# Two matmul blocks and an attention block on one core: gate and value of the last 1536 tokens by seven half-size products

## The chip, the cores and the metric

One core of a Trainium2 chip runs the whole program. The metric is device time in microseconds (us) of one execution; lower is better. The four compute engines are TensorE (PE in the profile), VectorE (DVE), ScalarE (ACT) and GpSimd (POOL); SyncE (SP) issues nearly all DMAs. Each engine works through its own instructions in order and waits for the others by semaphores.

## The reference

```python
kv = np.einsum('bhsd,bhse->bhde', k, v)          # q, k, v: 4 x 8 x 576 x 64
out = np.einsum('bhsd,bhde->bhse', q, kv)
x = out / np.sqrt(np.mean(out * out, -1) + 1e-6) * g_norm   # then 2304 tokens x 512
g = x @ w_gate                                    # 512 x 1536
x = (g / (1 + np.exp(-g)) * (x @ w_val)) @ w_out  # 1536 x 512
h = x @ w_in2                                     # 512 x 2048
out = (np.maximum(h, 0) + np.log1p(np.exp(-np.abs(h)))) @ w_out2   # 2048 x 512
```

All inputs and the output are float32.

## The kernel before

Every large product is made with split operands: a matrix is written as a high part (rounded to the matmul's own format, fp32r) plus a low part (the rest), and three matmuls, high by high, high by low, low by high, add up in PSUM (`passes`, L653 to L657). ACT makes the high part of a weight by a copy (`split_high`, L871; `split_high2`, L877), POOL the low part by a subtraction (`low`, L488 to L491), DVE both parts of activations.

Stage 1 (gate, value, product with `w_out`) runs over 6 chunks of 384 tokens and 12 groups f of 128 features: 72 steps k. In a step PE runs `up1(k)`, 12 matmuls of 384 columns for the gate and 12 for the value, and then `down1(k - 1)`, 12 matmuls into four accumulators. ACT makes the silu (L899) and DVE the product and its two parts (L1114, L1105, L1107). The 12 weight groups are loaded and split once, in steps 0 to 11, and stay in the `arena`. Stage 2 has 6 chunks and 16 groups; a step is 12 matmuls of 384 columns and 9 of 512, and ACT and DVE make the softplus.

Attention of batch 0 is done before stage 1; that of batches 1 to 3 lies inside stage 1, at steps that tables give: `KV_AT` names the step whose gate products are followed by the k-by-v products of the head pairs (b,0) and, after the value, (b,1), and two steps on those of pairs (b,2) and (b,3); `TILE_AT` names the steps at which a tile of 128 tokens is multiplied by them, one in every second step:

```python
KV_AT = {1: 4, 2: 17, 3: 30}
TILE_AT = {1: (6, 8, 10, 12, 14), 2: (19, 21, 23, 25, 27), 3: (32, 34, 36, 38, 40)}
```

For a tile (b,j), DVE turns q (`turn_q`), PE multiplies (L595), ACT squares (L819) and takes a root (L824, with a table load before and one after it), DVE normalizes (L1045). Then SP writes the tile to DRAM in 32-row blocks (L384, 4 DMAs, "keep"), waits until that has landed, and reads it back in another order (L389, "fetch"); two steps later DVE turns it (L1034). SP's queue also has the weight loads (`load_step1`, L397; `load_step2`, L413), the q blocks (`load_q_blocks`, L374, 16 DMAs for a batch) and the head pairs of k and v (`next_pair`, L347 and L349, 4 DMAs a pair). What stands behind a waiting DMA in SP's queue waits with it.

The stage 2 weights take the place of the stage 1 weights in the arena during the last 12 steps of stage 1: ACT copies the high part (L881) as soon as a slot is free and the raw data are there, POOL makes the low part, and only then SP may load the raw data of the group after the next (two raw buffers).

Of the kernel before, what the change touches and what calls it, by code (L numbers as in the profile page):

```python
# [49 lines left out]

LATE2 = NF2 - 3
# [12 lines left out]
STEPS1 = NCH * NF1  # L64
# [28 lines left out]
def program(nc, ctx, q, k, v, g_norm, w_gate, w_val, w_out, w_in2, w_out2, out):  # L93
# [66 lines left out]
    tail = [4 * NF2 * SLOT2]  # L160

    def step_buffer(name, dt=F32):
        tail[0] += 4 * CH
        assert tail[0] <= 4 * ARENA
        return sb(name, [P, CH], dt, over="arena", shift=tail[0] - 4 * CH)

    act_a2, act_u2 = [], []
    for n in range(RING2):
        act_a2.append(step_buffer(f"act_a2_{n}"))
        act_u2.append(step_buffer(f"act_u2_{n}"))  # L170
        if n == 0:
            tail[0] = 4 * (NF1 - 1) * SLOT1
# [167 lines left out]

    @block.sync
    def _(sp):
# [98 lines left out]
        for f in range(8, NF1):  # L441
            load_step1(f)
        for b in range(1, B):
            for j in range(3):
                turn_x(b, j)
            if b + 1 < B:
                next_pair(b + 1, 0)
                next_pair(b + 1, 1)
                sp.wait_ge(w_ready, low_count(NF1 - 1))
                for t in range(KT):  # L450
                    load_q_blocks(b + 1, t)
            for j in range(3, NT):
                turn_x(b, j)
            if b + 1 < B:
                next_pair(b + 1, 2)
                next_pair(b + 1, 3)
# [746 lines left out]
```

## Time and profile before

| | |
|---|---|
| median of 3 runs | 906.96 us (906.44 to 1482.94) |
| the profiled execution | 906.13 us, of which the span of the profile is 904.3 us |
| granted TensorE clock, mean | 0.999 |
| PE busy in the span | 896.2 us |

A step of stage 1 takes PE 6.24 us, and 72 of them with the attention between them make the first part of the span, to about 499 us; stage 2 follows. The profile's busy time of PE counts the pipelined ends of matmuls, so the pace of matmuls is read from the distance between their starts.

### The profile page before, as it was taken

To read this page: it belongs to the slowest core of one execution; us is meant where nothing else is said; L and a number is where in the kernel's file an instruction comes from. 1 tells how busy PE (TensorE), PEld (TensorE's weight loads), DVE (VectorE), ACT (ScalarE), POOL (GpSimd) and SP (SyncE) were. 2 spreads that over 40 slices of the span, in tenths; PEclk is the share of its full clock that TensorE was granted. 3 is DMA by queue.
4 is the path that set the end of the run, shared out by engine and by line. 5 is a ranking of instruction groups with operands and counts; after the bars stand their busy time and mean duration, and the time that the engine had idled before them with its cause. 6 is when DMAs were issued, how large, how long until landed. Compare 5 with 4: busy or idle time off the path is not lost.

```text
span 904.3 us, 13404 instructions
## 1 busy us (share of the span) xinstructions
PE 896.2 (99%) x5146; PEld 850.1 (94%) x5146; DVE 527.7 (58%) x1009; ACT 354.8 (39%) x615; POOL 80.0 (9%) x44
## 2 busy tenths in 40 slices
PE   8999999999999999999999999999999999999998
PEld 7999999999999999999999989998998998999987
DVE  3656642453254314224234888878878878878875
ACT  5616420342034201001232754554544644644553
POOL 4635000000000000000454000000000000000000
PEclk9999999999999999999999999999999999999999
DMA  9982342133111200000243000000000000000000
GB/s 277 215 208 82 87 77 54 47 93 71 53 37 45 73 1 1 1 1 1 71 138 119 1 1 1 35 0 0 35 0 0 35 0 0 35 0 0 36 1 35
DMA packets 81129, 44.38 MB, mean 49 GB/s; under 512 B 36672, under 2 KB 73664, under 8 KB 81088
## 3 DMA queue, kind: packets, MB, share of 16 engines
q1 hardware_dynamic: 80928, 43.80, 18.2%
q8 instruction: 30, 0.49, 0.2%
q14 instruction: 11, 0.09, 0.0%
q10 hardware_dynamic: 160, 0.00, 0.0%
HBM read 35.52 MB, written 8.26 MB: 48 GB/s over the span
## 4 chain that ended last, share of the span: by engine, by line
PE 98%; issue 0%; DMA 0%; DVE 0%; POOL 0%; ACT 0%; ACTq 0%; POOLq 0%; SPq 0%
PE bank L655 24%; PE bank L657 24%; PE bank L656 24%; PE bank L772 7%; PE bank L773 7%; PE bank L771 7%; PE bank L595 2%; PE bank L588 1%; PE bank L663 1%; PE bank L669 0%; PE bank L561 0%; DMA q<-in_q 0%; PE bank L578 0%; PE bank L550 0%; PE bank L571 0%
## 5 line engine op out<-in xcount | busy, mean ns | idle before, releaser
L655 PE MATMUL bank<-x_hi,arena 128*128 128x384 f32 x938 | 315.1, 336 | 0.0
L657 PE MATMUL bank<-x_hi,arena 128*128 128x384 f32 x938 | 314.6, 335 | 0.0
L656 PE MATMUL bank<-x_lo,arena 128*128 128x384 f32 x938 | 314.0, 335 | 0.0
L655 PEld LDWEIGHTS bank<-x_hi,arena 128*128 128x128 f32 x938 | 176.2, 188 | 4.4
L656 PEld LDWEIGHTS bank<-x_lo,arena 128*128 128x128 f32 x938 | 176.1, 188 | 3.8
L657 PEld LDWEIGHTS bank<-x_hi,arena 128*128 128x128 f32 x938 | 176.0, 188 | 0.0
L1114 DVE TENSOR_TENSOR act_a<-act_a,bank 128x384 f32<-128x384 f32 x72 | 39.9, 554 | 228.1 <-PE bank L657 225.1
L899 ACT ACTIVATE act_a<-bank 128x384 f32<-128x384 f32 x72 | 35.3, 491 | 244.2 <-PE bank L657 240.3
L919 ACT ACTIVATE act_a<-bank 128x384 f32<-128x384 f32 x96 | 47.3, 492 | 179.1 <-PE bank L657 179.1
L773 PE MATMUL bank<-arena,g_lo 128*128 128x512 f32 x288 | 113.8, 395 | 0.0
L772 PE MATMUL bank<-arena,g_hi 128*128 128x512 f32 x288 | 113.6, 395 | 0.0
L771 PE MATMUL bank<-arena,g_hi 128*128 128x512 f32 x288 | 112.0, 389 | 0.0
L1107 DVE TENSOR_TENSOR g_lo<-act_a,g_hi 128x384 fp32r<-128x384 f32 x168 | 104.4, 621 | 5.8
L491 POOL TENSOR_TENSOR arena<-stage,arena 128x1024 fp32r<-128x1024 f32 (+1 forms) x23 | 66.9, 2918 | 394.7 <-ACT arena L881 366.0
L655 PE MATMUL bank<-g_hi,arena 128*128 128x384 f32 x288 | 97.9, 340 | 0.0
L657 PE MATMUL bank<-g_hi,arena 128*128 128x384 f32 x288 | 96.3, 334 | 0.0
L656 PE MATMUL bank<-g_lo,arena 128*128 128x384 f32 x288 | 96.2, 334 | 0.0
L1132 DVE SCALAR_TENSOR_TENSOR act_c<-act_w,act_u 128x384 f32<-128x384 f32 x96 | 53.5, 557 | 57.3 <-ACT act_w L923 57.3
L1105 DVE CAST g_hi<-act_a 128x384 fp32r<-128x384 f32 x168 | 73.0, 435 | 7.6
L773 PEld LDWEIGHTS bank<-arena,g_lo 128*128 128x128 f32 x288 | 54.0, 188 | 11.5
L772 PEld LDWEIGHTS bank<-arena,g_hi 128*128 128x128 f32 x288 | 54.0, 187 | 9.3
L771 PEld LDWEIGHTS bank<-arena,g_hi 128*128 128x128 f32 x288 | 54.1, 188 | 8.8
(90 smaller groups left out, 838.7 us busy)
## 6 DMA issues: line engine op xcount, KB each, us to landing
stage<-in_moe_w_out SPq DMA_DIRECT2D x28, 256.0 KB, 3.6
out_dram<-out_stage SPq DMA_DIRECT2D x18, 256.0 KB, 2.0
k<-in_k SPq DMA_DIRECT2D x16, 256.0 KB, 3.2
v<-in_v SPq DMA_DIRECT2D x16, 256.0 KB, 3.2
stage<-in_moe_w_in SPq DMA_DIRECT2D x16, 256.0 KB, 2.8
xy<-in_q SPq DMA_DIRECT2D x48, 72.0 KB, 3.0
stage<-in_moe_w_gate SPq DMA_DIRECT2D x12, 256.0 KB, 3.8
stage<-in_moe_w_val SPq DMA_DIRECT2D x12, 256.0 KB, 4.1
```

The source lines that it names most:

```text
L491: nc.gpsimd.tensor_tensor(slot[:, size:2 * size], raw, slot[:, 0:size].bitcast(F32), ALU.subtract).then_inc(w_ready, 1)
L655: nc.tensor.matmul(ps, hi, rhs_hi, start=first, stop=False)
L656: nc.tensor.matmul(ps, hi, rhs_lo, start=False, stop=False)
L657: return nc.tensor.matmul(ps, lo, rhs_hi, start=False, stop=last)
L771: nc.tensor.matmul(acc_ps[t][:, :], g[0], w[0], start=(f == 0), stop=False)
L772: nc.tensor.matmul(acc_ps[t][:, :], g[0], w[1], start=False, stop=False)
L773: last = nc.tensor.matmul(acc_ps[t][:, :], g[1], w[0], start=False, stop=(f == NF2 - 1))
L919: nc.scalar.activation(a, hid_ps[f % RING2][:, 0:CH], ACT.Abs).then_inc(abs_ready, 1)
L1105: nc.vector.tensor_copy(hi, g).then_inc(g_hi_ready, 1)
L1107: nc.vector.tensor_tensor(lo, g, hi.bitcast(F32), ALU.subtract).then_inc(g_split, 1)
L1114: nc.vector.tensor_tensor(act_a[:, f % 2, :], act_a[:, f % 2, :], val_ps[:, 0:CH], ALU.mult).then_inc(g_ready, 1)
L1132: nc.vector.scalar_tensor_tensor(act_c[:, :], w, 1.0, u, ALU.subtract, ALU.subtract).then_inc(rest_ready, 1)
```

## The change

The first 24 steps (`PLAIN`, chunks 0 and 1, 768 tokens) stay as they were. The last 1536 tokens are cut in 3 chunks of 512 tokens, and the 12 groups in two sets of 6 (`SEG`). For a chunk and a group, x and the pair (w_gate, w_val) are read as 2 by 2 blocks, x in halves of 256 features by 256 tokens, the weights in halves of 256 features by gate and value, and the four result blocks (gate and value, early and late 256 tokens) are made of seven products P1, P6, P7, P5, P2, P4, P3 of half size instead of eight (the Winograd form of Strassen's scheme). A step q (36 of them) is `up7(q)`, 7 products of 6 matmuls with 256 columns, and `down7(q - 1)`, 12 matmuls with 512 columns. P1 shares bank 0 with P2, P6 bank 2 with P4, P7 bank 3 with P3: P2 waits until ACT has copied P1 out (`keep_p1`), P4 and P3 until DVE has added P6 and P7.

- DVE (`glu7`): 7 additions of 256 columns with PSUM, 2 multiplications of 256 columns in SBUF, a cast and a subtraction of 512 columns in a step.
- POOL (`weight_sums`, `weight_lows`): for each of the 12 groups 4 sums of 256 columns and 5 low parts (two of 384, three of 512 columns); for each of 5 makings of x (`x_sums`) 6 sums of 512 columns.
- ACT: for a group `weight_highs` (768 and 512 columns) and, a step later, `weight_sum_highs` (1024); for a making of x 7 copies of 512 columns (`x7_high`), to which DVE adds 7 low parts (`x7_low`). A making falls in the steps q = 5, 11, 23 and 29, and one before q = 0.
- SP: `load7(f)` loads the raw weights again, gate and value in two buffers, `w_out` in one: its load for group f+1 waits until POOL has made the low part of group f.
- The chunks' order is 0, 1, 2 with groups 0 to 5, then 2, 1, 0 with groups 6 to 11; the half sums of chunks 0 and 1 are kept by ACT and added by DVE (`add_y`).
- Attention of all batches now lies in the 24 plain steps, one tile in every step.
- 11 of the 16 groups of stage 2 weights are split in q = 31 to 35 (2, 2, 2, 3 and 2 of them, at the end of ACT's step), 5 in the first chunk of stage 2. The first x of stage 2 is split by DVE at the end of q = 32.

```diff
-STEPS1 = NCH * NF1
+NC1 = 2
+PLAIN = NC1 * NF1
+SEG = NF1 // 2
+CHUNK7 = (0, 1, 2, 2, 1, 0)
+STEPS7 = len(CHUNK7) * SEG
+HALF = 256
+CH7 = 2 * HALF
...
+HIGH7_AT = {21: 0, 22: 1, 23: 2, 24: 3, 25: 4, 26: 5, 38: 6, 39: 7, 40: 8, 41: 9, 42: 10, 43: 11}
...
-KV_AT = {1: 4, 2: 17, 3: 30}
-TILE_AT = {1: (6, 8, 10, 12, 14), 2: (19, 21, 23, 25, 27), 3: (32, 34, 36, 38, 40)}
+KV_AT = {1: 4, 2: 10, 3: 15}
+TILE_AT = {1: (6, 7, 8, 9, 10), 2: (12, 13, 14, 15, 16), 3: (17, 18, 19, 20, 21)}
...
+        def load7(f):
+
+            if f == 0:
+                sp.wait_ge(kv_done, B * KT)
+            if f >= 2:
+                sp.wait_ge(w7_ready, LOWS7 * (f - 1))
+            for i, w in enumerate((w_gate, w_val)):
...
+            if f:
+                sp.wait_ge(w7_ready, LOWS7 * (f - 1) + 3)
+            sp.dma_start(raw7_out[:, :], w_out[f * P:(f + 1) * P, :]).then_inc(raw7_out_loaded, 16)
...
+        keep_x(1, 2)
+        sp.wait_ge(w_ready, low_count(NF1 - 1))
+        load_q_blocks(2, 0)
+        load_q_blocks(2, 1)
+        fetch_x(1, 2)
...
+        fetch_x(3, 1)
+        load7(1)
+        for j in range(2, NT):
+            keep_x(3, j)
+            fetch_x(3, j)
+        for f in range(2, NF1):
+            load7(f)
...
+        def up7(q):
...
+            for p in range(SEVEN):
+                if i == 0 and segment != 3:
+                    pe.wait_ge(x7_ready, SEVEN * m + p + 1)
...
+                if p == P2:
+                    pe.wait_ge(p1_kept, q + 1)
+                if p == P4:
+                    pe.wait_ge(u2_ready, q + 1)
...
+        def weight_highs(f):
+
+            act.wait_ge(raw7_loaded[f % 2], 32 * (f // 2 + 1))
+            act.wait_ge(down_done, slot7_free(f))
+            nc.scalar.activation(w7_part(f, 0, 0, 3), raw7[:, f % 2, 2 * P:2 * KT * P], ACT.Copy).then_inc(w7_hi_ready, 1)
+            act.wait_ge(raw7_out_loaded, 16 * (f + 1))
+            nc.scalar.activation(slots7[:, f % SEG, OUT7:RAW7], raw7_out[:, :], ACT.Copy).then_inc(w7_hi_ready, 1)
...
+        for q in range(STEPS7):
+            k = PLAIN + q
+            keep_p1(q)
+            silu7(q)
...
+            if k - 1 in HIGH7_AT:
+                weight_sum_highs(HIGH7_AT[k - 1])
+            if k in HIGH7_AT:
+                weight_highs(HIGH7_AT[k])
+            for f in range(EARLY2):
+                if STEPS7 - SEG + under(f) + 1 == q:
                     split_high2(f)
```

On SP, here is the queue at attention batch 1 and the loads for batch 2, of the kernel before, from the write of tile (1,2). `in_q` are the q blocks, `in_k` and `in_v` a head pair, `x_kept_rows<-x_norm` a keep and `xy<-x_kept_rows` a fetch:

```order
L384 DMA x_kept_rows<-x_norm 32x4x128 [waits xn_ready]
L384 DMA x_kept_rows<-x_norm 32x4x128 x3
L389 DMA xy<-x_kept_rows 128x512 [waits x_kept,x_ready,xs_ready]
L347 DMA k_62<-in_k 128x2x256 [waits kv_done]
L349 DMA k_rest_64<-in_k 64x2x64
L347 DMA v_63<-in_v 128x2x256
L349 DMA v_rest_65<-in_v 64x2x64
L347 DMA k_66<-in_k 128x2x256 [waits kv_done]
L349 DMA k_rest_68<-in_k 64x2x64
L347 DMA v_67<-in_v 128x2x256
L349 DMA v_rest_69<-in_v 64x2x64
L374 DMA xy<-in_q 32x18x32 [waits w_ready]
```

And the same place of the changed kernel:

```order
L506 DMA xy<-in_q 32x18x32 [waits w_ready]
L506 DMA xy<-in_q 32x18x32 x7
L526 DMA xy<-x_kept_rows 128x512 [waits x_kept,xs_ready]
L516 DMA x_kept_rows<-x_norm_odd 32x4x128 [waits xn_ready]
L516 DMA x_kept_rows<-x_norm_odd 32x4x128 x3
L506 DMA xy<-in_q 32x18x32 x8
L526 DMA xy<-x_kept_rows 128x512 [waits x_kept,x_ready,xs_ready]
L516 DMA x_kept_rows<-x_norm 32x4x128 [waits xn_ready]
L516 DMA x_kept_rows<-x_norm 32x4x128
L479 DMA k_62<-in_k 128x2x256 [waits kv_done]
L481 DMA k_rest_64<-in_k 64x2x64
L479 DMA v_63<-in_v 128x2x256
```

The q blocks of batch 2, which wait for the low part of the last weight group, now stand ahead of the fetches of tiles (1,2) and (1,3) and ahead of the head pairs (2,2) and (2,3).

On ACT, here is the end of stage 1 of the kernel before: a silu of each step and the high parts of stage 2 weights between them:

```order
L899 ACTIVATE act_a<-bank 128x384 [waits gate_done]
L881 ACTIVATE arena<-stage_124 128x1024 [waits raw_loaded2_0,down_done]
L899 ACTIVATE act_a<-bank 128x384 [waits gate_done]
L881 ACTIVATE arena<-stage_124 128x1024 [waits raw_loaded2_1,down_done]
L881 ACTIVATE arena<-stage_124 128x1024 [waits raw_loaded2_0,down_done]
L899 ACTIVATE act_a<-bank 128x384 [waits gate_done]
```

And of the changed kernel, steps q = 34 and 35: `sum_a<-bank` is `keep_p1`, the two after it the silus:

```order
L1207 ACTIVATE sum_a<-bank 128x256 [waits g_ready,p_done]
L1212 ACTIVATE gated<-gated 128x256 [waits gate_late_ready]
L1217 ACTIVATE gated<-gated 128x256 [waits gate_early_ready]
L1172 ACTIVATE arena<-stage_145 128x1024 [waits raw_loaded2_0,down_done]
L1172 ACTIVATE arena<-stage_145 128x1024 [waits raw_loaded2_1,down_done]
L1172 ACTIVATE arena<-stage_145 128x1024 [waits raw_loaded2_0,down_done]
L1207 ACTIVATE sum_a<-bank 128x256 [waits g_ready,p_done]
```

Three copies that wait for loads now stand ahead of the `keep_p1` for which P2 waits.

## Rows read from the trace of the kernel before

**Rows 1.** The page: busy time of the engines, and the chain that ended last

```profile
PE 896.2 (99%) x5146; PEld 850.1 (94%) x5146; DVE 527.7 (58%) x1009; ACT 354.8 (39%) x615; POOL 80.0 (9%) x44
...
PE 98%; issue 0%; DMA 0%; DVE 0%; POOL 0%; ACT 0%; ACTq 0%; POOLq 0%; SPq 0%
```

**Rows 2.** Timeline of PE, stage 1: start us, us, engine, line, op

```profile
148.02 0.33 PE L655 MATMUL bank<-x_hi,arena 128*128 128x384 f32 x1
...
150.62 0.33 PE L655 MATMUL bank<-x_hi,arena 128*128 128x384 f32 x1
```

**Rows 3.** Timeline of PE, stage 2: nine matmuls of 512 columns

```profile
701.95 0.39 PE L771 MATMUL bank<-arena,g_hi 128*128 128x512 f32 x1
...
704.03 0.33 PE L655 MATMUL bank<-x_hi,arena 128*128 128x384 f32 x1
```

**Rows 4.** Timeline of PE's weight loads after a wait, and PE in an attention tile

```profile
301.40 0.19 PEld L655 LDWEIGHTS bank<-g_hi,arena 128*128 128x128 f32 x1 [0.17 <-issue]
301.51 0.19 PEld L656 LDWEIGHTS bank<-g_lo,arena 128*128 128x128 f32 x1
...
156.74 1.05 PE L595 MATMUL bank<-kv_blocks,q_t 128*128 128x128 f32 x8
```

**Rows 5.** Timeline of SP's queue, and DMA issues (KB each, us to landing)

```profile
107.28 0.59 SPq L347 DMA_DIRECT2D k<-in_k  x1
...
109.84 8.71 SPq L374 DMA_DIRECT2D xy<-in_q  x16
118.59 1.94 SPq L384 DMA_DIRECT2D x_kept_rows<-x_norm_odd  x4
121.94 0.34 SPq L389 DMA_DIRECT2D xy<-x_kept_rows  x1
...
v_rest<-in_v SPq DMA_DIRECT2D x12, 32.0 KB, 2.9
```

**Rows 6.** One tile, step 8, on DVE, ACT and SP

```profile
80.33 0.55 DVE L1114 TENSOR_TENSOR act_a<-act_a,bank 128x384 f32<-128x384 f32 x1 [0.75 <-PE bank L657]
83.27 1.47 ACT L874 ACTIVATE arena<-stage 128x1536 fp32r<-128x1536 f32 x1
84.42 1.75 SPq L384 DMA_DIRECT2D x_kept_rows<-x_norm_odd  x4
```

**Rows 7.** Groups by form, POOL: busy us, mean ns of one | idle before

```profile
L491 POOL TENSOR_TENSOR arena<-stage,arena 128x1536 fp32r<-128x1536 f32 x10 | 35.5, 3561 | 28.7 <-ACT arena L874 28.7
L491 POOL TENSOR_TENSOR arena<-stage,arena 128x1024 fp32r<-128x1024 f32 x13 | 31.4, 2423 | 366.0 <-ACT arena L881 366.0
L485 POOL TENSOR_TENSOR arena<-stage,arena 128x512 fp32r<-128x512 f32 x3 | 4.0, 1330 | 2.7 <-ACT arena L868 2.7
```

**Rows 8.** Timelines of SP and ACT, end of stage 1: a load and the copy waiting

```profile
457.21 0.38 SPq L413 DMA_DIRECT2D stage<-in_moe_w_in  x1
...
460.69 1.06 ACT L881 ACTIVATE arena<-stage 128x1024 fp32r<-128x1024 f32 x1 [3.20 <-DMA stage<-in_moe_w_out]
```

**Rows 9.** Timelines of POOL and DVE: a low part with POOL busy, and one without

```profile
71.45 7.09 POOL L491 TENSOR_TENSOR arena<-stage,arena 128x1536 fp32r<-128x1536 f32 x2 [9.38 <-ACT arena L874]
75.20 3.75 DVE L1107 TENSOR_TENSOR g_lo<-act_a,g_hi 128x384 fp32r<-128x384 f32 x1
81.31 0.56 DVE L1107 TENSOR_TENSOR g_lo<-act_a,g_hi 128x384 fp32r<-128x384 f32 x1
```

**Rows 10.** Groups by form, DVE, ACT and PE: busy us, mean ns of one | idle before

```profile
L1045 DVE TENSOR_TENSOR x_norm<-bank,sums 128x256 f32<-128x256 f32 x12 | 4.5, 420 | 0.2
L868 ACT ACTIVATE arena<-stage 128x512 fp32r<-128x512 f32 x3 | 1.9, 620 | 0.0
L521 PE MATMUL bank<-ident 128*128 128x128 f32 x18 | 4.0, 397 | 2.0 <-POOL ident L479 2.0
```

**Rows 11.** Stretches: us, busy (x) of each engine, PEclk the granted clock

```profile
900.00:902.00 2.00, 0.65 (x3) 0.19 (x2) 0.00 (x0) 1.20 (x2) 0.00 (x0) 1.00 0.52 203
902.00:904.00 2.00, 0.00 (x0) 0.00 (x0) 0.00 (x0) 0.00 (x0) 0.00 (x0) 0.74 0.50 191
```

More of the change, by code:

```diff
@@ L156, in program @@
     q_rows0 = [sb(f"q_rows0_{n}", [P, J, P], F32, over="k_0", shift=4 * n * J * P) for n in range(2)]
[L160 to L172, printed above, removed]
@@ new lines, in program, with step_buffer @@
+    slots2 = [RING7 + f * SLOT2 if f < EARLY2 else (f - EARLY2) * SLOT2 for f in range(NF2)]
+    step_places = ([4 * (NF2 - EARLY2) * SLOT2 + 4 * n * CH for n in range(8)]
+                   + [4 * (RING7 + EARLY2 * SLOT2) + 4 * n * CH for n in range(2)])
+    assert step_places[7] + 4 * CH <= 4 * RING7 and step_places[9] + 4 * CH <= 4 * ARENA
+    def step_buffer(name, n, dt=F32):
+        return sb(name, [P, CH], dt, over="arena", shift=step_places[n])
+    act_a2 = [step_buffer(f"act_a2_{n}", n) for n in range(RING2)]
@@ L440, in _ @@
         next_pair(1, 3)
-        for f in range(8, NF1):
+        for f in range(8, NF1 - 1):
             load_step1(f)
[L443 to L456, printed above, removed]
+        next_pair(2, 0)
+        next_pair(2, 1)
+        keep_x(1, 0)
+        load_step1(NF1 - 1)
+        fetch_x(1, 0)
+        keep_x(1, 1)
+        fetch_x(1, 1)
+        keep_x(1, 2)
[3 more added lines that the diff above has]
+        fetch_x(1, 2)
+        keep_x(1, 3)
+        load_q_blocks(2, 2)
+        load_q_blocks(2, 3)
+        fetch_x(1, 3)
+        keep_x(1, 4)
+        next_pair(2, 2)
+        next_pair(2, 3)
+        fetch_x(1, 4)
+        keep_x(2, 0)
+        next_pair(3, 0)
+        fetch_x(2, 0)
+        keep_x(2, 1)
+        next_pair(3, 1)
+        fetch_x(2, 1)
+        keep_x(2, 2)
+        load_q_blocks(3, 0)
+        load_q_blocks(3, 1)
+        fetch_x(2, 2)
+        keep_x(2, 3)
+        load_q_blocks(3, 2)
+        load_q_blocks(3, 3)
+        next_pair(3, 2)
+        next_pair(3, 3)
+        fetch_x(2, 3)
+        keep_x(2, 4)
+        fetch_x(2, 4)
+        load7(0)
+        keep_x(3, 0)
+        fetch_x(3, 0)
+        keep_x(3, 1)
+        fetch_x(3, 1)
[5 more added lines that the diff above has]
+            load7(f)
         for f in range(NF2):
@@ L516, in _ @@
+        x_sums(0)
+        for f in range(SEG):
+            weight_sums(f)
+            weight_lows(f)
+        x_sums(1)
+        x_sums(2)
+        for f in range(SEG, NF1):
+            weight_sums(f)
+            weight_lows(f)
+        x_sums(3)
+        x_sums(4)
+        for f in range(NF2):
+            wait_slot2(pool, f)
+            low(high_count2(f), arena[:, slots2[f]:slots2[f] + SLOT2], stage2[:, f % 2, :], RAW2)
     @block.tensor
@@ new lines, in down7 @@
+        def down7(q):
+            segment, i = divmod(q, SEG)
+            f = (segment // 3) * SEG + i
+            pe.wait_ge(g_split, PLAIN + q + 1)
+            fresh = i == 0 and segment != 3
+            ends = i == SEG - 1 and segment != 2
+            if fresh:
+                pe.wait_ge(acc_free, 1 + NC1 + (segment if segment < 3 else segment - 1))
+            for t in range(KT):
+                last = passes(acc_ps[t][:, :], w7_out(f, 0, t), w7_out(f, 1, t), g7_hi[:, q % 2, :], g7_lo[:, q % 2, :],
+                              fresh, ends)
+                if ends and t < KT - 1:
+                    last.then_inc(acc_done, 1)
+            last.then_inc(down_done, 1)
@@ L782, in _ @@
         up1_first()
-        for k in range(1, STEPS1):
+        for k in range(1, PLAIN):
             if k <= 2:
@@ L788, in _ @@
             down1(k - 1)
-        down1(STEPS1 - 1)
-        pe.wait_ge(silu_ready, STEPS1)
+        up7(0)
+        down1(PLAIN - 1)
+        for q in range(1, STEPS7):
+            up7(q)
+            down7(q - 1)
+        down7(STEPS7 - 1)
         for f in range(LAG2):
@@ L946, in _ @@
         split_high(2)
-        for k in range(1, STEPS1):
+        for k in range(1, PLAIN):
             silu(k)
@@ L1030, in turn_x @@
         def turn_x(b, j):
-            before = sum(1 for i in range(NT) if i % 3 == j % 3) * (b - 1) + j // 3
-            dve.wait_ge(x_back[j % 3], 16 * (before + 1))
+            n = number(b, j)
+            dve.wait_ge(x_back[n % 3], 16 * (n // 3 + 1))
             nc.vector.transpose(x_place(b, j), x_blocks(b, j)).then_inc(x_ready, 1)
```

430 lines of the change are left out of this document (366 added, 64 removed).

## The prediction

> **What bounds the kernel now.** I read the page first: PE is busy 99% of the span and is 98% of the chain that ended last, POOL is busy for 80.0 us of 904.3 [rows 1]. The kernel is bound by PE from end to end, so a change wins what it takes off PE's own work and loses every microsecond in which PE waits. Then I read PE's pace from the timeline. In stage 1, 15 matmuls of 384 columns start within 150.62 - 148.02 = 2.60 us, 173.3 ns each [rows 2]. In stage 2, nine of 512 columns take 704.03 - 701.95 = 2.08 us, 231.1 ns each [rows 3]. Both are 0.4514 ns a column, so a matmul has no fixed cost of its own here. Last I read the queues that the change loads more, SP, ACT, POOL and DVE, for what they can deliver in a step.
>
> **PE's own work.** A step of 36 matmuls takes 36 x 0.1733 = 6.24 us; the 48 steps replaced take 299.5 us. A new step has 42 matmuls of 256 columns. At 0.4514 ns a column each takes 115.6 ns, if its weights are there: after a wait the second load starts 0.11 us after the first [rows 4], so a load takes 0.11 us and just fits. A step is 42 x 0.1156 + 12 x 0.2311 = 4.86 + 2.77 = 7.63 us, 36 of them 274.7 us: 24.8 us less. Bounds: as little as 0.110 us (the load alone) would give 1512 x 0.0056 = 8.5 us more; if the near tie of load and stream cost 5 ns a matmul, as between 0.1156 and 0.120, it would give 6.6 us less. A product that takes as long as one of 384 columns is excluded, since neither its load nor its stream takes so long. I take 24.8.
>
> The Trainium skill, "TensorE: Matmul & The Clock Gate", section "Back-to-back issue gap", gives N/2.4 + 2.5 ns for N columns. That would be 109 ns for 256 columns and 162.5 for 384; the trace has 173.3 for 384 and disagrees, so the sum does not use it. By the page alone the new steps would win 18.7 us (48 x 36 x 0.1625 less 36 x (42 x 0.1092 + 12 x 0.2158)).
>
> **Attention in 24 steps: SP is late.** V(k) is the end of step k's value products. A tile adds 0.89 us to PE's step (8 matmuls in 1.05 with their ends [rows 4]), so steps with tiles are 7.13 us apart. The normalized tile is there 4.1 us after V (84.42 - 80.33), and ACT's weight copy starts 2.9 us after V [rows 6]. SP issues a q block in 8.71/16 = 0.54 us, a k or v piece in (109.84 - 107.28)/4 = 0.64, a keep in 1.8, a fetch in 0.34, and a piece lands 2.9 us after its issue [rows 5].
>
> Batch 2: the q blocks wait for the low part of weight group 11. ACT copies group 11 in step 9, from V(9)+2.9 to +4.4, POOL needs 3.56 [rows 7]: V(9)+8.0, or V(10)+0.9. Behind it stand 8 q blocks (4.4), a fetch (0.3), a keep (1.8), 8 q blocks (4.4), a fetch (0.3), a half keep (0.9) and 8 pieces of k and v (5.1), 17.2 in all; the last lands near V(10)+20. PE reaches its products after the gate of step 12: tile 0.89, down 2.08, step 11 6.24, gate 2.08, at V(10)+11.3, and the pair before takes 0.9. PE waits 8 us. The same sum for batch 3 (keep 1.8, q 4.4, pairs 5.1 from V(15)+4.1, landing at +17.8, against V(15)+13.1) gives 4.6.
>
> Steps 21 to 23: `load7(1)` waits in SP's queue for the low part of `w_out` of group 0, whose high part ACT makes only at the end of step 21. Behind it stand the keeps of tiles (3,2) to (3,4), and DVE's normalize of step 21 waits for the first. ACT V+4.4, POOL two low parts of 384 and one of 512 +3.4, SP 0.5, keep 3.2 to its landing, normalize 0.8, then the fetch 2.7 and the turn 0.7: V(21)+15.7. Only then comes the glu of step 22, for which the value of step 23 waits; PE gets there at V(21)+11.1. I count 4.6. Attention together: 17.2 us, with ends at 9 (SP without the pieces' queueing) and 21.
>
> **Weights: POOL is slower than PE.** POOL takes 0.20 us + 2.19 ns a column (512: 1.33, 1024: 2.42, 1536: 3.56 [rows 7]): 0.76 for 256, 1.04 for 384. A group is 4 x 0.76 + 2 x 1.04 + 3 x 1.33 = 9.1 us, against 7.63 of PE. POOL and DVE also hold each other up: the DVE subtraction of 384 columns took 3.75 us instead of 0.56 while POOL made two low parts, until the second ended [rows 9]. DVE has four such instructions in a step (operands in SBUF only), about 1.3 us of holding; a group then takes 10.4. I take the middle, 9.75.
>
> Does PE feel it? `w_out` has one raw buffer: group f+1 is loaded after POOL's third low part of f, and ACT gets it some 3.2 us later (457.21 to 460.69 for two DMAs [rows 8]), copies 0.62 [rows 10], and only then does `keep_p1`, 0.4, of the next step. P2 can start 4 x 6 x 0.1156 = 2.78 us into its step and must wait for that. So PE runs at POOL's pace as long as ACT takes groups: steps q = 0 to 3 and 17 to 20 (before, POOL has a lead). 8 x (9.75 - 7.63) = 17.0 us, ends 8 x 1.5 = 11.8 and 8 x 2.8 = 22.2.
>
> The Trainium skill, "SBUF — State Buffer", section on the shared port pair, says the pair is an exclusive lock held for a whole instruction. The 3.75 us agrees. With the full lock the term would be the upper end, 22.2.
>
> **Makings of x.** Seven low parts of 512 columns, some 0.7 us each, are 5 us more for DVE around one step, beside its 5.1 (nine instructions of 0.42 [rows 10], a cast and a subtraction). Two come before, three within and two after. The last, for which P3 waits, ends some 1.3 us after P3 could start. Four makings: 5.2 us, ends 0 and 7. The one in the plain steps is covered by PE's 6.24.
>
> **The way into stage 2.** At the end of q = 34 ACT makes three high parts. The third needs the raw buffer of the first: high 1.06, POOL 2.42, load and wait 3.5, high 1.06, keep_p1 0.4, begun when `down7(33)` ends, 0.3 us into q = 35: 8.7 us, where P2 wanted it at 2.8. PE waits 6.0 us. In the kernel before, ACT waits the same way [rows 8], but only the silu is behind it. The split of x at the end of q = 32 has 8 DVE instructions on SBUF beside POOL's 2.42 us low parts; two of them held up cost 5 us in q = 33 if all meet, I take half, 2.5. Together 8.5, ends 3 and 11. The other work (kept half sums, `add_y`, 5 late groups) lies beside `down7` or two steps ahead and costs nothing, up to 1.5 if that cover is gone.
>
> **Sum.** -24.8 + 17.2 + 17.0 + 5.2 + 8.5 = +23.1 us on the profiled execution's 906.1 (0.8 less than the median): 929.2 us, 2.5% slower. A measurement tells about 2% from no change.
>
> **Rivals.**
> - A, not slower: the queues keep up. One mechanism, in SP and ACT: the k and v pieces land before V(10)+12.2 and the `w_out` copy ends before P1's end plus 1.9 us, so PE never waits for either. Then 34.2 us go away: 895.0; with x and stage 2 also covered 881.3. For it: DMA engines are far from full and loads land in 3 us. Against: the issue times are rows, and POOL's 9.1 is above 7.63 without any contention. It decides if SP runs 8 us ahead of my sum. Down to 888, faster than 2%, it takes nearly all terms at their low end.
> - B, about the same: the pace of the groups is POOL's bare 9.1 or hidden by its lead, and attention costs half: 906.1 - 24.8 + 9 + 11.8 + 3 + 3 = 908.1.
> - C, the clock: after the last matmul the granted clock was still 1.00 up to 902 and a mean 0.74 from 902 to 904 [rows 11], PE having ended at 900.7. PE's waits of over 4 us (four by my sum) may drop it in the same way. Price: the 18 idle products at the start took 4.0 us [rows 10], twice their later pace, 2 us lost; four times that on top: 937.2. The Trainium skill, the page on TensorE above, section "HAM oscillation", names this loss for kernels with waits in their loop; it would make C the case.
>
> **Chances.** The forecast with C (above 925.0) 0.57, of which C 0.15; B and rival A down to 888.8 0.32; faster 0.11. The likeliest case by itself has 915 to 943. The range reaches to B and A's 900 and to C: 903 to 945.
>
> **What would show it.** Right: PE idle for 5 us or more after the gate of step 12 with DMA k or v as its releaser, PE waits at P2 for ACT L1207 of 1 to 3 us in q = 0 to 3 and 17 to 20 and of about 6 in q = 35, ACT waiting for `in_moe_w_out`, DVE subtractions of over 1 us beside POOL, and PE idle of some 48 us more. Wrong: a pace of 256 columns other than 0.1156 us, PE busy above 98% again, or waits at other places.

## The result, and the profile after

The changed kernel takes 952.61 us, median of 4 runs (950.52 to 953.43), against 907.34 us of the kernel before; ratio 1.050, 95% interval 1.0476 to 1.0522. It is slower, by twice what was forecast, and outside the range. Below, a ratio is turned into microseconds on 907 (0.001 is 0.9 us), since the kernel before was timed again beside each set of experiments.

The page of the changed kernel, busy time and the chain that ended last, for [rows 1]:

```profile
PE 897.7 (94%) x5362; PEld 827.4 (87%) x5362; DVE 678.0 (71%) x1284; ACT 423.1 (44%) x742; POOL 241.4 (25%) x185
...
PE 74%; POOL 7%; DVE 7%; issue 4%; SPq 3%; DMA 3%; ACT 2%; DVEq 0%; POOLq 0%; ACTq 0%
```

PE was 98% of the chain and is 74%. The busy time of PE hardly moved and says little: ends are modelled, and matmuls at a lower clock count as busy. What PE waited for (waits of the changed kernel: total us, times, longest us):

```profile
PE bank L901 <- ACT sum_a L1207: 15.5, 8, 5.5
PE bank L834 <- DMA v_rest<-in_v: 11.8, 4, 5.1
PE bank L901 <- DVE sum_b L1535: 5.1, 2, 4.1
PE bank L901 <- DVE act_a L1507: 4.7, 1, 4.7
PE bank L901 <- DVE ring L1520: 4.6, 6, 0.9
PE bank L1058 <- DVE g_lo L1500: 2.3, 3, 1.1
```

The same view of the kernel before has only waits of the start, 2.0 us and less. By place these six rows are: `keep_p1` late for P2, in q = 35 (5.5) and in seven other steps, six of them while weight groups are made (10.0 together, 0.4 of it in q = 33); pieces of k and v at steps 12 and 17; P4 of q = 33, on the way into stage 2 (4.1), and P4 of q = 5, behind a making of x (1.0); the value of step 23; x not yet split; and one that was not forecast, early stage 2.

The windows of the changed kernel; the columns are those of [rows 11], PEclk is the granted clock:

```profile
100.00:150.00 50.00, 43.25 (x295) 40.36 (x294) 23.01 (x50) 18.02 (x26) 0.00 (x0) 0.90 0.52 121
150.00:200.00 50.00, 43.84 (x286) 42.66 (x285) 29.23 (x60) 26.30 (x35) 11.04 (x10) 0.93 0.44 110
200.00:250.00 50.00, 41.77 (x252) 40.04 (x251) 26.61 (x49) 22.27 (x36) 38.01 (x38) 0.90 0.33 90
250.00:350.00 100.00, 96.70 (x656) 89.11 (x655) 77.84 (x156) 31.84 (x64) 34.15 (x30) 1.00 0.05 17
350.00:450.00 100.00, 91.81 (x625) 84.38 (x624) 79.20 (x135) 32.63 (x61) 65.34 (x58) 1.00 0.15 46
500.00:550.00 50.00, 39.96 (x219) 36.36 (x218) 28.72 (x53) 17.28 (x26) 23.02 (x10) 0.86 0.34 109
```

The kernel before has 1.00 in all of them. In four stretches of 50 us the mean clock is 0.86 to 0.93, and they hold the long waits. Seen closer, around the value products of step 23, on PE:

```profile
212.64 0.34 PE L903 MATMUL bank<-x_hi,arena 128*128 128x384 f32 x1
217.72 0.69 PE L901 MATMUL bank<-x_hi,arena 128*128 128x384 f32 x1 [4.74 <-DVE act_a L1507]
```

and the windows of that place:

```profile
216.00:218.00 2.00, 0.28 (x1) 0.29 (x2) 1.97 (x4) 0.00 (x0) 2.00 (x2) 0.50 0.33 35
218.00:220.00 2.00, 2.00 (x7) 2.00 (x8) 1.97 (x2) 0.00 (x0) 2.00 (x3) 0.50 0.49 164
224.00:226.00 2.00, 2.00 (x18) 2.00 (x17) 0.00 (x0) 1.40 (x3) 1.45 (x3) 1.00 1.00 315
```

In the second row PE starts 6 matmuls in 2 us, 0.32 us apart, where at full clock it starts 11; the clock is at its lower level, 1.2 GHz, from 216.0, within the wait, to 222.8, and from the end of the wait on PE is "busy" all the while. There are six such stretches in this kernel, 41 us in all, at step 12, step 17, step 23 and in q = 2, 33 and 35, each at a wait of 2.8 to 5.5 us. The other waits, of 2.3 us and less, have none of their own. That is no threshold: in the experiments below some waits of 1.8 us have one. By the distances between their starts, the matmuls in them took 11.4 us longer than at the usual pace.

### The profile page after: what moved, and what is told of

Same layout as the page of the kernel before. It is cut to its first block, busy times and chain, and to the rows that moved or that the text cites. A ratio compares the mean times of both kernels' runs of the same rounds, so it can differ in the third digit from the quotient of the medians.

```text
span 951.6 us, 14670 instructions
## 1 busy us (share of the span) xinstructions
PE 897.7 (94%) x5362; PEld 827.4 (87%) x5362; DVE 678.0 (71%) x1284; ACT 423.1 (44%) x742; POOL 241.4 (25%) x185
## 3 DMA queue, kind: packets, MB, share of 16 engines
q1 hardware_dynamic: 95328, 53.23, 20.6%
## 4 chain that ended last, share of the span: by engine, by line
PE 74%; POOL 7%; DVE 7%; issue 4%; SPq 3%; DMA 3%; ACT 2%; DVEq 0%; POOLq 0%; ACTq 0%
PE bank L901 17%; PE bank L903 16%; PE bank L902 16%; PE bank L1060 7%; PE bank L1059 7%; PE bank L1058 7%; POOL slots L719 2%; SPq L506 1%; POOL slots L711 1%; PE bank L841 1%; POOL slots L715 1%; PE bank L834 1%; PE bank L909 1%; DMA v_rest<-in_v 1%; SPq L516 1%
## 5 line engine op out<-in xcount | busy, mean ns | idle before, releaser
L901 PE MATMUL bank<-x_hi,arena 128*128 128x384 f32 x554 | 189.6, 342 | 5.2 <-DVE act_a L1507 4.7
L903 PE MATMUL bank<-x_hi,arena 128*128 128x384 f32 x554 | 188.6, 341 | 0.0
L902 PE MATMUL bank<-x_lo,arena 128*128 128x384 f32 x554 | 187.9, 339 | 0.0
L901 PE MATMUL bank<-ring,slots 128*128 128x256 f32 x504 | 146.8, 291 | 25.9 <-ACT sum_a L1207 15.5
L903 PE MATMUL bank<-ring,slots 128*128 128x256 f32 x504 | 144.4, 287 | 0.0
L902 PE MATMUL bank<-ring,slots 128*128 128x256 f32 x504 | 144.4, 286 | 0.0
L1274 ACT ACTIVATE act_a<-bank 128x384 f32<-128x384 f32 x96 | 47.2, 492 | 177.1 <-PE bank L903 177.1
L901 PEld LDWEIGHTS bank<-ring,slots 128*128 128x128 f32 x504 | 98.2, 195 | 31.8 <-ACT sum_a L1207 17.1
L901 PEld LDWEIGHTS bank<-x_hi,arena 128*128 128x128 f32 x554 | 105.8, 191 | 10.7 <-DVE act_a L1507 5.1
L902 PEld LDWEIGHTS bank<-x_lo,arena 128*128 128x128 f32 x554 | 105.5, 190 | 3.4
L903 PEld LDWEIGHTS bank<-x_hi,arena 128*128 128x128 f32 x554 | 105.4, 190 | 0.0
L673 POOL TENSOR_TENSOR arena<-stage,arena 128x1024 fp32r<-128x1024 f32 (+1 forms) x26 | 74.3, 2869 | 104.3 <-ACT arena L1172 71.0
L902 PEld LDWEIGHTS bank<-ring,slots 128*128 128x128 f32 x504 | 98.4, 195 | 1.3
L903 PEld LDWEIGHTS bank<-ring,slots 128*128 128x128 f32 x504 | 98.4, 195 | 0.0
L1594 DVE SCALAR_TENSOR_TENSOR act_c<-act_w,act_u 128x384 f32<-128x384 f32 x96 | 55.6, 580 | 51.4 <-ACT act_w L1278 51.4
L1500 DVE TENSOR_TENSOR g_lo<-act_a,g_hi 128x384 fp32r<-128x384 f32 x120 | 73.2, 610 | 4.2
```

Source lines behind the costliest of these rows:

```text
L673: nc.gpsimd.tensor_tensor(slot[:, size:2 * size], raw, slot[:, 0:size].bitcast(F32), ALU.subtract).then_inc(w_ready, 1)
L901: nc.tensor.matmul(ps, hi, rhs_hi, start=first, stop=False)
L902: nc.tensor.matmul(ps, hi, rhs_lo, start=False, stop=False)
L903: return nc.tensor.matmul(ps, lo, rhs_hi, start=False, stop=last)
L1274: nc.scalar.activation(a, hid_ps[f % RING2][:, 0:CH], ACT.Abs).then_inc(abs_ready, 1)
L1500: nc.vector.tensor_tensor(lo, g, hi.bitcast(F32), ALU.subtract).then_inc(g_split, 1)
```

## The experiments

### Attention alone

The kernel before with nothing changed but the tables and SP's order:

```diff
-KV_AT = {1: 4, 2: 17, 3: 30}
-TILE_AT = {1: (6, 8, 10, 12, 14), 2: (19, 21, 23, 25, 27), 3: (32, 34, 36, 38, 40)}
+KV_AT = {1: 4, 2: 10, 3: 15}
+TILE_AT = {1: (6, 7, 8, 9, 10), 2: (12, 13, 14, 15, 16), 3: (17, 18, 19, 20, 21)}
```

> The kernel before with only the attention tables and the SP queue order of the changed kernel: one token tile in every step, all tiles in steps 6 to 21, no seven products. Theory 1 (SP's queue is late by itself): PE waits after the gate of step 12 for about 5.5 + 0.9 us and in step 17 for about 2.7 + 4.1 us, as in the changed kernel, and the clock falls to its lower level for some 17 us in all, which costs 5 us more: 907.3 + 13.2 + 5 = 925. Rival 2 (those waits come from the new work on ACT, DVE and POOL in the same steps, as the first making of x): the waits are under 2 us in all and the time is 907 to 910.

Measured: 927.1 us, ratio 1.0207 (1.0183 to 1.0231), 18.8 us slower. It was expected at 925. Its waits have one main row, and PE at step 12 reads as in the changed kernel:

```profile
PE bank L628 <- DMA v_rest<-in_v: 12.0, 4, 5.1
PE bank L569 <- POOL q_rows L538: 2.3, 1, 2.3
...
118.42 1.12 PE L628 MATMUL bank<-v,k 128*64 128x64 f32 x16 [5.06 <-DMA v_rest<-in_v]
```

So the denser attention costs its part with no seven products in the program: 12.0 us of waits for k and v, and 20.6 us at the lower clock in two stretches, at steps 12 and 17. The profiled execution, the slowest of the four, has a third stretch, from 9.3 to 16.2, around a wait of 2.3 us at the start (1.0 in the kernel before). Where the 5 us come from stands in SP's queue of the changed kernel:

```profile
97.10 5.39 SPq L506 DMA_DIRECT2D xy<-in_q  x8
...
105.00 4.30 SPq L506 DMA_DIRECT2D xy<-in_q  x8
...
110.84 0.48 SPq L479 DMA_DIRECT2D k<-in_k  x1
...
112.65 0.61 SPq L481 DMA_DIRECT2D v_rest<-in_v  x1
```

PE stood from 111 on, when the first of these pieces had just been issued; 9.7 us of q blocks stand ahead of it.

### q blocks issued by ACT

```diff
+Q_ON_ACT = {11: ((2, 2), (2, 3)), 13: ((3, 0),), 14: ((3, 1),), 15: ((3, 2),), 16: ((3, 3),)}
...
+            silu(k)
+            if k in Q_ON_ACT:
+                act.wait_ge(w_ready, low_count(NF1 - 1))
+                for b, t in Q_ON_ACT[k]:
+                    act_load_q(b, t)
```

> The changed kernel with half of the q blocks of batch 2 and all of batch 3 issued from ACT's queue in steps 11 and 13 to 16, so that SP's queue loses 4.4 and 8.7 us of issuing. Theory 1 (SP's issue time makes the waits of steps 12 and 17): the wait of step 12 falls from 6.3 to 1 to 3 us, that of step 17 from 6.7 to under 1, two stretches of low clock go, and the time falls by 12 to 17 us, to 936 to 941. Rival 2 (the DMAs' landing or the chain over DRAM is what is late): both waits stay within 1.5 us of what they were, 949 to 953. Rival 3 (ACT becomes late instead): gaps before silus, and less than 5 us won.

Measured: 943.45 us, ratio 1.0393 (1.0373 to 1.0413), 9.6 us less than the changed kernel. On PE:

```profile
113.15 0.69 PE L831 MATMUL bank<-v,k 128*64 128x64 f32 x16 [2.91 <-DMA v_rest<-in_v]
...
208.50 0.69 PE L898 MATMUL bank<-x_hi,arena 128*128 128x384 f32 x1 [5.94 <-DVE act_a L1515]
```

The waits for k and v fell from 11.8 to 4.2 us, so their cause is SP's issue time; at step 12 3.9 us of them are left, with a stretch at the lower clock, more than expected, and the time is 2.5 us above the range of theory 1. The wait at step 23 grew from 4.7 to 5.9. It has another cause and took a little of the gain.

### Dummy products in the waits

Both kernels put matmuls whose result nobody reads (or that add zero) into PE's longest waits, to keep PE active there without moving anything.

```diff
+                    fill(FILL_KV.get(b, (0, 0))[0])
                     pair(b, 2)
...
+            fill(FILL_VALUE.get(k, 0))
             pe.wait_ge(g_ready, k)
```

> The changed kernel, and in six places where PE waits for long (step 12, step 17 twice, value of step 23, q = 33 before P4, q = 35 before P2) PE makes dummy products of 128 columns that nobody reads, each set some 0.3 to 0.7 us shorter than the wait. Theory 1 (the clock's fall is a cost of its own): the granted clock stays at its upper level but for the stretch near 247 us, and the time falls by 8 to 11 us, to 942 to 945. Rival 2 (the stretches at the lower level lie mostly in the waits and cost nothing): within 2 us of 952.6.

Measured: 965.68 us, 13 us slower than without. The fill at step 12 of this kernel, on PE:

```profile
110.05 9.99 PE L772 MATMUL bank<-ident 128*128 128x128 f32 x88
```

44 matmuls were asked for, 88 are recorded: these operands are plain float32, not fp32r, and each was executed as two of 0.11 us. The fills outlasted the waits, and the time left the range of both theories. The run says nothing of the clock's price; the next has half the counts.

> The changed kernel with dummy products put into the five longest waits of PE, half as many as in fill_waits because each was executed as two matmuls there. Nothing else is changed, so every wait keeps its end. Theory 1 (after a wait of 2.5 to 6 us the clock stays at its lower level for another 3.4 to 10 us, which costs the changed kernel some 11 us over its waits): lower level nearly gone, 942 to 946 us. Rival (the lower clock is not caused by the waits, or the matmuls issued in it would have been late anyway): 950 to 953 us.

Measured: 948.47 us, ratio 1.0464 (1.0446 to 1.0481), 3.2 us less. The two intervals still touch, but every run of it (947.60 to 949.76) is below every run of the changed kernel. It lies between the two theories. Its windows, for those above:

```profile
100.00:150.00 50.00, 48.39 (x358) 45.73 (x357) 24.99 (x54) 20.09 (x28) 1.84 (x2) 1.00 0.58 131
200.00:250.00 50.00, 43.54 (x278) 41.46 (x278) 24.98 (x46) 21.23 (x35) 40.58 (x41) 0.93 0.32 92
500.00:550.00 50.00, 48.98 (x327) 45.50 (x326) 32.85 (x58) 21.88 (x35) 25.09 (x11) 1.00 0.36 112
```

The cause holds: with PE active in the waits the clock stays at 2.4 GHz. Two stretches are left, at waits that were not filled: q = 2 (3.5 us of wait, 6.8 at the lower clock) and, new here, q = 20 (1.8 us of wait, 3.4 at the lower clock). The price doesn't hold. Of the 11.4 us 7.4 went, but the time fell by 3 to 5. Comparing the same product's start in both profiles, 4.6 us were won on the way into stage 2 and 2.7 at step 12; some 2 were given back by q = 2 and 1.7 at q = 20. There PE follows the weight groups, and where it follows another engine, a faster PE only waits longer.

### The weight groups

First the high part of `w_out`, for which ACT waited ahead of `keep_p1`, was put one step later, behind it:

```diff
             keep_p1(q)
             silu7(q)
+            if k - 1 in HIGH7_AT:
+                weight_out_high(HIGH7_AT[k - 1])
```

> The changed kernel with the high part of w_out of a weight group made one step later, behind keep_p1 in ACT's order; nothing else moves. Theory 1 (P2 waits only because keep_p1 stands behind a copy that waits for its DMA): the waits of 1.5 to 1.8 us in q = 17 to 20 go, and that of 3.0 us in q = 1 becomes under 1; 9 to 11 us less, 942 to 944, the 3.4 us at the lower clock in q = 1 included. Rival 2 (POOL's pace of 9.6 us a group binds anyway): PE waits at the start of up7 for w7_ready instead and less than 3 us are won, 950 or more.

Measured: 951.05 us, ratio 1.0486 (1.0467 to 1.0505), not told apart from the changed kernel. The waits for `keep_p1` fell from 15.5 to 11.2 us, those for DVE's `sum_b` rose from 5.1 to 7.3: the 2.8 us of q = 2 are gone, and 3.4 us stand at P4 of q = 5 instead. That is the rival in its time, though PE does not wait where the rival said. Then the single raw buffer was taken away: raw `w_out` goes into the place of its own low part.

```diff
-            if f:
-                sp.wait_ge(w7_ready, LOWS7 * (f - 1) + 3)
-            sp.dma_start(raw7_out[:, :], w_out[f * P:(f + 1) * P, :]).then_inc(raw7_out_loaded, 16)
+            sp.wait_ge(down_done, slot7_free(f))
+            sp.dma_start(out_raw(f), w_out[f * P:(f + 1) * P, :]).then_inc(raw7_out_loaded[f % 2], 16)
```

> The changed kernel with the raw w_out of a group loaded into the place of its low part (the low part is made in place), so that the one raw buffer, and the round trip through it, is gone, and with it the DMA that held up SP's queue in steps 21 to 23. POOL's work is the same. Theory 1 (the round trip and the queue cause the waits at value 23, q = 1 and q = 17 to 20, and POOL's slower pace alone is covered by its lead of four steps): those 15 us and one stretch of lower clock go, 934 to 940 us. Rival (POOL's pace of 9.6 us against 7.8 binds whatever the buffers): the waits move to later steps, 947 to 952 us.

Measured: 946.22 us, ratio 1.0432 (1.0397 to 1.0466), 6.1 us less, between the two theories. The wait at step 23 is gone, q = 17 to 19 have 0.5 us of wait left and q = 20 has 2.1, but q = 1 has 1.8 and a new one of 4.8 stands in q = 5. (By the count of `keep_p1` the waits that my expectations put at q = 1 and 19 lie in q = 2 and 20.) POOL, DVE and PE of this kernel at q = 5:

```profile
248.95 0.93 POOL L701 TENSOR_TENSOR slots_sums<-raw 128x256 f32<-128x256 f32 x1
...
258.46 1.47 POOL L735 TENSOR_TENSOR ring_sums<-xy 128x512 f32<-128x512 f32 x1
...
263.27 2.88 DVE L1522 SCALAR_TENSOR_TENSOR ring<-xy,gain,ring 128x256 fp32r<-128x256 f32 x2
...
268.20 0.58 PE L903 MATMUL bank<-ring,slots 128*128 128x256 f32 x1 [4.78 <-DVE sum_b L1537]
```

A group took POOL 258.46 - 248.95 = 9.51 us with no wait in it, against 7.78 us of a step. After six groups the lead was used up, the sums of x came late, and their DVE work held `glu7` up.

The waits of 1.8 us in q = 1 (it ends at 227.71) and of 2.1 us in q = 20 each have a stretch of 3.4 us at the lower clock, though in the changed kernel four waits of 1.3 to 1.6 us in q = 17 to 20 have none:

```profile
227.00:229.00 2.00, 1.29 (x10) 1.29 (x11) 1.24 (x4) 0.66 (x2) 2.00 (x3) 1.00 0.00 0
229.00:231.00 2.00, 2.00 (x11) 2.00 (x10) 1.12 (x5) 0.84 (x2) 2.00 (x3) 0.51 0.00 1
```

So the groups were begun earlier (0 and 1 by two steps, the others by one; the load of group 2 stands ahead of the last keep):

```diff
-HIGH7_AT = {21: 0, 22: 1, 23: 2, 24: 3, 25: 4, 26: 5, 38: 6, 39: 7, 40: 8, 41: 9, 42: 10, 43: 11}
+HIGH7_AT = {19: 0, 20: 1, 22: 2, 23: 3, 24: 4, 25: 5, 37: 6, 38: 7, 39: 8, 40: 9, 41: 10, 42: 11}
```

> out_in_slot (946.2 us, ratio 1.043) with the weight groups begun earlier: groups 0 and 1 two steps, all others of both sets one step. In out_in_slot POOL made a group in 9.54 us against 7.78 us of a step of PE, ran out of its lead in the sixth group, and its sums of x then held up DVE (wait of 4.9 us at P4 of q = 5, 2.3 us at q = 19). Theory 1 (POOL's pace costs only what its lead does not cover): the waits at value 23, q = 1, 3, 5, 19 and a stretch or two of lower clock go, 932 to 937 us. Rival (POOL and DVE hold each other up in the making of x wherever the groups stand): the wait at q = 5 stays within 1 us of 4.9, 942 to 946 us.

Measured: 939.3 us, ratio 1.0355 (1.0336 to 1.0375), 7.0 us less again, though 2 above the expected range. The wait at q = 5 is gone and the clock from 200 to 250 is 1.00. The second set paid for it: at its new place ACT stands first for the slot and then for the landing of `w_out`, ahead of `keep_p1`, and PE waits some 0.7 us in each of q = 14 to 19:

```profile
331.75 0.85 ACT L1183 ACTIVATE slots<-raw 128x768 fp32r<-128x768 f32 x1 [2.58 <-PE bank L907]
334.31 0.63 ACT L1185 ACTIVATE slots<-slots_sums 128x512 fp32r<-128x512 f32 x1 [1.71 <-DMA slots_sums<-in_moe_w_out]
334.84 0.37 ACT L1211 ACTIVATE sum_a<-bank 128x256 f32<-128x256 f32 x1
```

### The way into stage 2

```diff
+HIGH2_LATER = (8, 10)
...
-            if q == 5 * SEG + 2:
...
-                split_x(NC1, bass.ds(0, CB), val_done, PLAIN, scaled=False, to=(x2_hi, x2_lo))
+            if 5 * SEG < q <= 5 * SEG + KT:
...
+                split_x(NC1, bass.ds(0, CB), val_done, PLAIN, scaled=False, to=(x2_hi, x2_lo), parts=(t,))
```

> The changed kernel with the way into stage 2 spread out: the split of x of stage 2 is made one quarter a step in q = 31 to 34 instead of whole at the end of q = 32, and the third high part of q = 34 stands behind keep_p1 of q = 35. Theory 1 (these two placements cause the waits of 4.4 us at P4 of q = 33 and 5.8 us at P2 of q = 35 and their two stretches of lower clock of 6.8 us): 937 to 942 us. Rival (POOL is busy with low parts all through these steps, so DVE's instructions are held up wherever they stand, and ACT waits for the same buffer later): waits of 1 to 2 us at four steps instead, 945 to 950 us.

Measured: 939.28 us, ratio 1.0361 (1.0341 to 1.0382), 12.5 us less, as theory 1 said. Between 505 and 565 the two profiles part by 13.0 us; they part by 2.0 before, at the start and up to q = 5, where the edit changes nothing. What was removed, in the changed kernel: DVE at the end of q = 32, then ACT between q = 34 and 35.

```profile
504.15 2.83 DVE L1481 TENSOR_TENSOR x_lo<-xy,x_hi 128x384 fp32r<-128x384 f32 x1
506.91 2.51 DVE L1479 CAST x_hi<-xy 128x384 fp32r<-128x384 f32 x1
...
532.81 1.06 ACT L1172 ACTIVATE arena<-stage 128x1024 fp32r<-128x1024 f32 x1 [4.14 <-DMA stage<-in_moe_w_out]
533.77 0.37 ACT L1207 ACTIVATE sum_a<-bank 128x256 f32<-128x256 f32 x1
```

Two DVE instructions that take 0.56 and 0.35 us beside an idle POOL took 2.83 and 2.51 beside its low parts. One rearrangement removed the two waits, 9.7 us, for a new one of 0.7 in q = 34, and two stretches of lower clock.

### Widths of matmuls

```diff
+        for columns, rows in ((256, 128), (256, 64), (128, 128), (192, 128), (320, 128), (256, 128)):
+            for n in range(42):
```

> The kernel before with 252 matmuls behind its last product, 42 each in this order: 256 columns with 128-column weights, 256 with 64-column weights, 128 with 128, 192 with 128, 320 with 128, 256 with 128, each with its own weight load. Theory 1 (a 256-column product with new weights is bound by the load of 128 weight columns, 0.12 us): 120 ns for the first and last row, 115.6 ns with 64-column weights, still 110 to 120 ns at 192 and 128 columns, 144.5 ns at 320. Rival (a fixed cost of a few ns for a matmul of this width): 120 ns with 64-column weights too, and 90 ns or less at 192 columns. If the clock falls in the rows, all are twice as long and are compared with each other.

First starts of four of the rows on PE, and of the last (x2: the first two of 42 are drawn together):

```profile
900.82 0.40 PE L809 MATMUL bank<-x_lo,x_hi 128*128 128x256 f32 x2
...
905.85 0.40 PE L809 MATMUL bank<-x_lo,x_hi 128*64 128x256 f32 x2
...
910.50 0.28 PE L809 MATMUL bank<-x_lo 128*64 128x256 f32 x1
```

(905.85 - 900.82)/42 = 119.8 ns a matmul with 128 columns of weights; with 64 it is (910.50 - 905.85)/41 = 113.4. By the same reckoning 128 and 192 columns took 110.4 and 112.5 ns, 320 took 147.1, and 256 at the end 119.8 again, all at clock 1.00. So with a fresh load of 128 weight columns there is a floor of about 110 ns, and at 256 columns 4 ns are lost on the 115.6 of the stream's rate, 6 on what 64 weight columns take. Theory 1 holds in its main point, since fewer weight columns make the product faster; the floor is lower than the expected 120. That the loss comes from floor and stream being so close is the likeliest reading and not shown.

### Together

`together` is q_on_act, out_in_slot and late_groups in one. `together2` adds the earlier groups and all q blocks of batch 2 on ACT. `together3` puts the high parts of the second set behind `keep_p1`.

> The changed kernel with three edits at once: half of the q blocks of batch 2 and all of batch 3 issued from ACT, the raw w_out in the place of the low part, and the way into stage 2 spread out. If the three causes are separate their gains add: 952.6 - 9.2 - 15 - 12 = 916 us, 912 to 922. If they share what binds (POOL's pace, or DVE), it ends at 928 to 938. In no case is it expected below 908, the kernel before being at 907.

> together (925.3 us, ratio 1.021) with the earlier groups of early_groups and with the first half of the q blocks of batch 2 issued by ACT too, at the end of step 10. If the remaining waits at step 12 (3.1 us), value 23, q = 1, 3 and 19 (1.3 to 4.9 us) and the three stretches of lower clock go: 925.3 - 3.1 - 11.1 - 4 = 907 us, 905 to 911, which is the time of the kernel before; what is then left over the gain of 18 us on PE's own work is the five makings of x, the entry of stage 2 and the tile work. If ACT, now with 24 to 32 more issues, becomes late for silu or P1: 915 to 925 us.

> together2 (915.75 us, ratio 1.010) with the highs of the second set of weight groups placed behind keep_p1 of the next step. In together2 ACT stood at the end of the step waiting for the slot and then 1.7 us for the w_out load to land, and PE waited 0.8 to 1.2 us for keep_p1 in six steps, 5.5 us in all. Theory 1 (only this placement causes them; 1.5 us of copies fit between keep_p1 and the silu): 910 us, 908 to 912, still not below the 906.5 us of the kernel before. Rival (POOL's group then starts 2 us later and its lead runs out at the sixth group, as in out_in_slot, with 2 to 5 us of wait at q = 19 or 20): 913 to 917 us.

Measured: 925.3 us, ratio 1.0210 (1.0193 to 1.0227); 915.75, ratio 1.0103 (1.0086 to 1.0120); 914.08, ratio 1.0076 (1.0059 to 1.0094). The separate gains sum to 9.6 + 6.1 + 12.5 = 28.2 us, and `together` has 26.2: the causes are nearly separate. It still missed the 912 to 922 expected, which counted 15 us for `out_in_slot`, where 6.1 came. `together2` missed its range by 5 us, and lies in that of its rival, ACT late for P1: I had not counted the new waits of the second set. `together3` is hardly faster, as its rival said: the six waits became two of 1.5 us. PE of this kernel in q = 19 and 20:

```profile
364.87 0.38 PE L905 MATMUL bank<-ring,slots 128*128 128x256 f32 x1 [1.49 <-ACT sum_a L1211]
...
374.38 0.39 PE L905 MATMUL bank<-ring,slots 128*128 128x256 f32 x1 [1.48 <-ACT sum_a L1211]
```

No version beat the kernel before; the best is 6.9 us (0.8%) slower. Of the 45 us lost, 38 are accounted for by changes that take a cause away. In `together3` 17.8 us of waits are left that the kernel before hasn't (5.8 for `keep_p1`, 4.6 and 1.4 for parts of x, 3.7 for k and v, 2.3 in early stage 2), nearly all that the seven products save, and one stretch at the lower clock.

## Why the prediction was right or wrong

The direction and nearly every place were right, the size was not: +23.1 us was forecast, +45.3 measured. Term by term, waits by the rows above:

| term | forecast, us | measured, us |
|---|---|---|
| PE's own work | -24.8 | -18.4 |
| step 12; step 17; value of step 23 | 8; 4.6; 4.6 | 5.7; 6.2; 4.7 |
| weight groups | 17.0 | 10.0 |
| makings of x | 5.2 | 6.3 |
| q = 35; q = 33 | 6.0; 2.5 | 5.5; 4.1 |
| early stage 2 | 0 | 2.3 |
| all waits | 47.9 | 44.8 |
| matmuls at the lower clock | 0 | 11.4 |

- **The rate of 256 columns was mis-sized.** I took the stream's 115.6 ns because a load "just fits". 1512 x 4.2 ns = 6.4 us. The text had 0.120 as a bound; a near tie should have been priced at it. [Rows 4] gave 0.11 us for a load, and the run gives 110 ns. The rate comes from that run; in the changed kernel itself an undisturbed step takes 7.78 us against the 7.63 summed, which makes the term -19.4. The prediction also has a slip in its estimate from the formula of the Trainium skill, "TensorE: Matmul & The Clock Gate", section "Back-to-back issue gap": with the figures given there the new steps would win 22.5 us, not 18.7.
- **Attention** was right in sum (16.6 against 17.2) and mechanism, shown for steps 12 and 17 by the run of it alone and by q_on_act, for step 23 by out_in_slot. That the sum fits is in part luck: one place came out lower, another higher. SP issued step 12's pieces earlier than I summed. At step 17 both pairs were waited for (2.33 and 3.83 us), where I counted one.
- **Weight groups: the pace was right, the claim of who feels it was not.** POOL's 9.63 us a group (9.75 forecast) is there. But I charged it in all eight steps; waits came in q = 1 and 2 (0.7 and 2.8 us) and in q = 17 to 20, none in q = 0 and 3. It is a lead that is used up, not a toll: begun earlier, the same pace costs less. The single raw buffer was a part of it (up to 4 us of ACT's waiting in a group of the second set, q = 17 for one), not all, as act_out and out_in_slot show together.
- **The way into stage 2**: the places and ACT's wait for the load are as forecast. For q = 33 I had halved "two held up cost 5 us if all meet"; they met.
- **Makings of x** came out near the forecast, but no run took them away, so what they cost is read from the waits alone.
- **Early stage 2 was missed**, and not tested either: DVE's `softplus` beside the late low parts (2.78 us for one of 0.56 at 557.37) costs 2.3 us, though I had said that they cost nothing.
- **The clock was the failed step.** It stood as rival C at 0.15, priced at 8 us, and at nothing in the sum, though my own sum had four waits of over 4 us and [rows 11] showed the clock below 1.00 right behind PE's last work. It is no rival to the forecast but a consequence of it. Six stretches came, not four, one of them behind a wait of 2.8 us; a stretch cost 1.9 us of matmul time (11.4/6) where C had priced 2, so it was their number and their place in the sum that were wrong. The waits made them: fill_half has the same order of work and no stretch where it fills. Their price on the path is less sure than their length, 11.4 us at most: filling gave 3 to 5 back, since much of it lay where PE followed another engine.

Those rows add to 906.1 - 18.4 + 44.8 + 11.4 = 943.9; the profiled execution took 953.4. Most of the 9.5 us left is at the edges of waits. From 212.64 to 217.72 are 5.08 us between starts, of which the profile puts 4.74 down as wait and 0.17 are the pace: another 0.17 are lost, which the profile counts as the busy end of the last matmul. And the second matmul after a wait comes 0.22 us after the first, not 0.12:

```profile
370.89 0.39 PE L901 MATMUL bank<-ring,slots 128*128 128x256 f32 x1 [1.30 <-ACT sum_a L1207]
371.11 0.28 PE L902 MATMUL bank<-ring,slots 128*128 128x256 f32 x1
371.23 0.28 PE L903 MATMUL bank<-ring,slots 128*128 128x256 f32 x1
```

That is about 0.27 us a wait, some 7 us over the 27 waits that the kernel before hasn't. The prediction had no such term. The rest wasn't taken apart.

The Trainium skill, "TensorE: Matmul & The Clock Gate", section "HAM oscillation", says that waits inside a kernel throw the clock back, so that work behind them runs cold. The trace agrees, at 0.50 behind the wait of 4.74 us. The same section of the Trainium skill counts the whole excess of the cold time as lost. Here 7.4 us of excess were removed and 3 to 5 us came back.

Rival A fell with the waits for k and v in SP's queue, rival B with the same and with the groups' 10 us.

## What to carry to other kernels

A kernel that is bound by one engine to 98% has no room for "a little late": list the waits a change brings, and then add what they bring themselves, a quarter of a microsecond at each one's edges and the lower clock, in the sum and not as a rival. An algorithm that saves an eighth of the products (18 us of 907 here) pays in additions on the other engines and in loads; here those broke a schedule in four places, and removing the causes brought back 38 of 45 us and still no gain. When the operation that takes over a bottleneck comes within a few per cent of another limit (here a load and a stream of 0.11 and 0.116 us), measure it or take the worse.

## What the runs showed of the hardware that I had not expected

- 256-column products with a fresh 128-column weight load take 119.8 ns each, with 64 weight columns 113.4; at 128 and 192 columns about 110 to 112.
- The second of two matmuls after a wait started 0.10 us later than the pace (0.22 us against 0.12, q = 17).
- A plain float32 matmul of 128 columns was executed as two recorded matmuls of 0.11 us each; those with fp32r operands are one.
- At a wait of 2.8 us (q = 2) the clock was at its lower level for 3.4 us, at one of 4.74 for 6.8. At waits of 1.8 us it was so for 3.4 us in out_in_slot (q = 1) and in fill_half (q = 20), at one of 1.6 us in the changed kernel (q = 20) not. At its lower level a 256-column matmul takes 0.213 us instead of 0.120.
